# Three stages of attention, soft MoE and an output MLP on one core: first loads, last pair's outputs, last w2, and the first chunk of the last stage in another order

## The reference

```python
q_pool = q.reshape(B, H, S // 2, 2, D).mean(axis=3)          # 576 queries of each head
scores = scale * q_pool @ k.T ; attn = softmax(scores) ; x = attn @ v
...
logits = x @ phi                                              # x (2304, 512), phi (512, 32)
d = softmax over tokens ; slot_input = d.T @ x                # 8 experts, 4 slots each
h = np.maximum(slot_input[e] @ w1[e], 0.0) ; slot_out[e] = h @ w2[e]
x = softmax_over_slots(logits) @ slot_out
...
h = x @ w_in ; g = h - np.tanh(h) ; out = g @ w_out           # w_in (512, 2048), w_out (2048, 512)
```

## Time and profile before

| | us |
|---|---|
| median of 3 runs (lowest to highest) | 835.5 (834.91 to 835.62) |
| the profiled execution's own time | 835.48 |
| its span in the trace | 833.7 |
| PE busy in the span | 789.9 (95%) |
| DVE, ACT, POOL busy | 521.4, 504.1, 248.7 |

### The profile page before, as it was taken

The page is one execution under the profiler, slowest core; times in us unless marked ns, Lnnn a source line. Parts: engine busy times, 40 slices in busy tenths (PEclk is TensorE's granted clock), DMA queues, the critical chain, the costliest instruction groups (busy, mean ns, idle before and its releaser), DMA issues. The chain is left out here.

```text
span 833.7 us, 16574 instructions
## 1 busy us (share of the span) xinstructions
PE 789.9 (95%) x5819; PEld 596.7 (72%) x5819; DVE 521.4 (63%) x988; ACT 504.1 (60%) x878; POOL 248.7 (30%) x156
## 2 busy tenths in 40 slices
PE   4899999999999999999999998888879999999998
PEld 3777777777777777777777775644348888888886
DVE  3666766766766766766776674520076766667673
ACT  3676676676676676676666755311196666666662
POOL 2304304404404404403403300000086343434342
PEclk8999999999999999999999999899999999999999
DMA  6453303303303303303303175289920000000000
GB/s 142 145 147 86 84 4 87 85 0 85 85 0 85 85 0 85 85 0 85 85 0 86 65 268 206 98 328 396 387 101 26 13 13 25 25 25 25 25 25 25
DMA packets 83728, 75.49 MB, mean 91 GB/s; under 512 B 42480, under 2 KB 60912, under 8 KB 83696
## 3 DMA queue, kind: packets, MB, share of 16 engines
q1 hardware_dynamic: 81360, 74.47, 27.9%
q10 hardware_dynamic: 2336, 0.59, 0.4%
HBM read 70.32 MB, written 4.72 MB: 90 GB/s over the span
## 5 line engine op out<-in xcount | busy, mean ns | idle before, releaser
L535 ACT ACTIVATE prob<-ps,neg_max 128x512 f32<-128x512 f32 (+1 forms) x144 | 141.5, 983 | 146.7 <-DVE spare L442 145.5
L321 PE MATMUL ps<-ident,prob 128*128 128x128 f32 x1296 | 164.7, 279 | 11.3 <-ACT prob L535 9.3
L321 PEld LDWEIGHTS ps<-ident,prob 128*128 128x128 f32 x1296 | 141.2, 142 | 37.9 <-ACT prob L535 31.5
L337 PE MATMUL ps<-probT,v_nat 128*64 128x256 f32 (+1 forms) x1152 | 153.6, 411 | 0.0
L438 DVE TENSOR_REDUCE part_neg<-ps 128x1 f32<-128x512 f32 x160 | 109.3, 692 | 49.2 <-PE ps L276 41.6
L412 DVE COPY probT<-ps 128x128 f32<-128x128 f32 (+1 forms) x208 | 86.7, 442 | 66.8 <-PE ps L321 63.2
L211 POOL TENSOR_TENSOR kT<-k_raw,ones 128x1152 fp32r<-128x1152 f32 x15 | 31.6, 2107 | 295.1 <-ACT k_raw L507 295.1
L507 ACT ACTIVATE probT<-ps 128x512 f32<-128x512 f32 x192 | 106.3, 602 | 21.8 <-PE ps L321 21.3
L337 PEld LDWEIGHTS ps<-probT,v_nat 128*64 128x64 f32 x1152 | 77.1, 136 | 50.9 <-issue 3.2
L276 PE MATMUL ps<-kT,qT_hi 64*128 64x512 f32 (+1 forms) x768 | 109.0, 360 | 2.4 <-DVE qT_lo L429 2.4
L1042 PE MATMUL ps<-w_hi,g_even 128*128 128x512 f32 x320 | 102.7, 392 | 2.2 <-POOL g_even L1132 2.1
(11 more groups left out here) (155 smaller groups left out, 1106.0 us busy)
## 6 DMA issues: line engine op xcount, KB each, us to landing
slot<-in_moe_w SPq DMA_DIRECT2D x16, 2048.0 KB, 13.0
v_nat<-in_v SPq DMA_DIRECT2D x16, 576.0 KB, 5.0
k_nat<-in_k SPq DMA_DIRECT2D x30, 288.0 KB, 4.1
q_nat<-in_q SPq DMA_DIRECT2D x32, 256.0 KB, 4.2
out<-res SPq DMA_DIRECT2D x18, 256.0 KB, 2.0
slot<-in_moe_w_in SPq DMA_DIRECT2D x4, 1024.0 KB, 15.6
slot<-in_moe_w_out SPq DMA_DIRECT2D x8, 512.0 KB, 11.7
q_nat_r<-in_q SPq DMA_DIRECT2D x32, 32.0 KB, 3.5
```

The lines of the kernel that those rows point to most:

```text
L321: last = nc.tensor.transpose(dst[:, n * P:(n + 1) * P], prob[h][:, kt * P:(kt + 1) * P], ident[:])
L337: last = nc.tensor.matmul(ps[64 * h:64 * h + D, VBANK, 0:n], v_nat[par][:, h, kt, :], probT[g][:, kt, h, :], start=(kt == 0), stop=(kt == ...
L535: nc.scalar.activation(prob[h][:, 0:first], row[:, 0:first], ACT.Exp, bias=neg_max[:, j:j + 1], scale=-1.0, accum_out=sums).then_inc(exp_b ...
```

## The change

Five edits, here with the lines that matter.

First pair's loads: each of the two queues, SP and ACT, issues one k DMA and then one q DMA.

```diff
+                first = isinstance(n, int) and n == 0
+                wait(sp, ktr_full, n * 2)
+                load_k(sp, n, (0,) if first else (0, 1))
                 wait(sp, q_sum, 2 * n)
...
+                load_q(sp, n, (0,) if first else (0, 1))
                 sp.wait_ge(rest_zero, 1)
...
-            load_k(act, 0)
+            load_k(act, 0, (1,))
+            load_q(act, 0, (1,))
```

```diff
+            def last_pv(p, par):
+                pe.wait_ge(first_evac, tiles_of(p, ROUNDS))
+                pv(p, par, 1, 0, 8, False)
+                pe.wait_ge(second_a, (p + 1) * ROUNDS)
+                pe.wait_ge(second_b, doubles_of(p, ROUNDS))
+                pv(p, par, 1, 8, 16)
+                pe.wait_ge(third_evac, tiles_of(p, ROUNDS))
+                pv(p, par, 1, 16, 18)
...
                 if last:
-                    wait(pe, first_evac, tiles_of(p, ROUNDS))
-                    turn_out(p, 0)
-                    pv(p, par, 1, 0, len(PV_ORDER))
-                    pe.wait_ge(out_evac, p * 2 + 1)
+                    pe.wait_ge(first_evac, tiles_of(p, ROUNDS) - 1)
+                    turn_out(p, 0, 0)
+                    last_pv(p, par)
                     turn_out(p, 1)
...
+                    if last and r == ROUNDS - 1:
+                        empty_v(dve, nc.vector.tensor_copy, p, 0)
...
-                    empty_v(p, 0)
-                    empty_v(p, 1)
+                    empty_v(act, copy, p, 1)
```

```diff
-                for q in (1, 3):
-                    part = u4[q * NS:(q + 1) * NS, n * BANK:(n + 1) * BANK]
-                    ins = nc.vector.tensor_tensor(part, ps[q * NS:(q + 1) * NS, u_bank(n), :], part.bitcast(F32), ALU.subtract)
-                ins.then_inc(u_lo, 1)
+                part = u4[P // 2:P, n * BANK:(n + 1) * BANK]
+                nc.vector.tensor_tensor(part, ps[P // 2:P, u_bank(n), :], part.bitcast(F32), ALU.subtract).then_inc(u_lo, 1)
...
+                    if e == E - 1 and f % (FTE // len(last_w2)) == 0:
+                        pe.wait_ge(last_w2[f // (FTE // len(last_w2))], 16)
```

```diff
-                        for n in ((0, 1), (2,), (3,), ())[b]:
-                            u_high(n)
-                            if n == 0:
-                                for k in (0, 1, 2):
-                                    w_high(k)
+                        if b == 0:
+                            u_high(0)
+                            w_high(0)
+                            u_high(1)
+                        elif b == 1:
+                            u_high(2)
...
+                    if is_first(c) and b:
+                        high(c, par, b - 1)
+                        if b == 1:
+                            u_high(3)
...
-                        for k in ((3,), (4, 5), (6, 7), ())[b]:
+                        for k in ((1,), (2, 3), (4, 5), (6, 7))[b]:
                             w_high(k)
...
-                        for n in ((0, 1, 2, 3), (4, 5), (), (6, 7))[b]:
+                        for n in ((0, 1), (2,), (4,), (6,))[b]:
                             w_low(n)
...
-                        for n in ((0, 1), (2,), (3,), ())[b]:
+                        for n in ((0, 1), (2, 3), (), ())[b]:
                             u_low(n)
...
+                    if is_first(c) and b:
+                        w_low(2 * b + 1)
...
-                pe.wait_ge(gl_done, c * BLOCKS + b + 1)
+                block = range(b * FB, (b + 1) * FB)
+                both_high_first = is_first(c)
                 pe.wait_ge(gh_done, c * BLOCKS + b + 1)
...
+                    for ft in block:
+                        product(par, i, ft, g_hi, w_hi)
...
+                        product(par, i, ft, g_hi, w_lo)
+                    if not both_high_first:
+                        project_low(c, par, b, i)
+                if both_high_first:
+                    for i in range(TPC):
+                        project_low(c, par, b, i)
```

More of the change, by code:

```diff
@@ L131, in attention, with load_k, load_q @@
         block = ctx.enter_context(nc.Block())
-        def load_k(eng, n):
-            for h in range(2):
+        def load_k(eng, n, heads=(0, 1)):
+            for h in heads:
                 eng.dma_start(k_nat[:, :, h, :], k_src[:, bass.ds(n * 2 + h, 1), :].rearrange("p o (t d) -> p (o t) d", d=D)).then_inc(k_in, 16)
+        def load_q(eng, n, heads=(0, 1)):
+            for h in heads:
+                eng.dma_start(q_nat[:, h].rearrange("p t a d -> p t (a d)"), q_main[:, bass.ds(n * 2 + h, 1)].rearrange("p o t e -> p (o t) e")).then_inc(q_in, 16)
         @block.sync
@@ L322, in turn_prob, with pv @@
                     last.then_inc(ptr_full, 1)
-            def pv(p, par, g, lo, hi):
+            def last_pv(p, par):
[6 more added lines that the diff above has]
+                pv(p, par, 1, 16, 18)
+            def pv(p, par, g, lo, hi, whole=True):
                 n = GN[g]
@@ L328, in pv @@
                     wait(pe, pv_evac, p * 2 + g)
+                if lo == 0 and whole:
                     rounds = MIX + 1 if g == 0 else ROUNDS
@@ L412, in evac, with empty_v @@
             return copy(probT[g][:, k0:k1, h, col:col + P], src.rearrange("p (c q) -> p c q", c=n))
+        def empty_v(eng, copy, p, g):
+            eng.wait_ge(pv_done, p * 2 + g + 1)
+            wait(eng, otr_full, p * 2 + g - 1)
+            copy(outT[g][:], ps[:, VBANK, 0:GN[g]]).then_inc(pv_evac, 1)
         def group_free(eng, p, r):
@@ L549, in body @@
                     if r == 0 and not first:
-                        empty_v(p - 1, 0)
+                        empty_v(act, copy, p - 1, 0)
                     for h in range(heads_of(r)):
@@ L565, in body @@
                     if r == MIX - 1 and not first:
-                        empty_v(p - 1, 1)
+                        empty_v(act, copy, p - 1, 1)
                     if r != MIX:
@@ L1028, in hidden, with product @@
                 last.then_inc(m_full, 1)
+            def product(par, i, ft, a, w, stop=False):
+                return nc.tensor.matmul(ps[:, 2 * HB + i, :], a[par][:, ft * CW + i * P:ft * CW + (i + 1) * P], w(ft),
+                                        start=(ft == 0 and a is g_hi and w is w_hi), stop=stop)
             def project(c, par, b):
-                pe.wait_ge(gl_done, c * BLOCKS + b + 1)
+                block = range(b * FB, (b + 1) * FB)
+                both_high_first = is_first(c)
                 pe.wait_ge(gh_done, c * BLOCKS + b + 1)
@@ L1037, in project, with project_low @@
                         wait(pe, o_evac[i], c)
-                    for ft in range(b * FB, (b + 1) * FB):
+                    for ft in block:
+                        product(par, i, ft, g_hi, w_hi)
                         if i == 0 and ft % PF == 0:
-                            pe.wait_ge(wl_done, ft // PF + 1)
-                        for k, (a, w) in enumerate(((g_hi, w_hi), (g_hi, w_lo), (g_lo, w_hi))):
-                            last = nc.tensor.matmul(ps[:, 2 * HB + i, :], a[par][:, ft * CW + i * P:ft * CW + (i + 1) * P], w(ft),
-                                                    start=(ft == 0 and k == 0), stop=(ft == FT - 1 and k == 2))
-                    if b == BLOCKS - 1:
-                        last.then_inc(o_full, 1)
+                            n = ft // PF
+                            if n % 2 and n > 1:
+                                pe.wait_ge(wl_dve, n // 2)
+                            else:
+                                pe.wait_ge(wl_pool, n // 2 + 1 + (n > 0))
+                        product(par, i, ft, g_hi, w_lo)
[4 more added lines that the diff above has]
+                        project_low(c, par, b, i)
+            def project_low(c, par, b, i):
+                if i == 0:
+                    pe.wait_ge(gl_done, c * BLOCKS + b + 1)
+                for ft in range(b * FB, (b + 1) * FB):
+                    last = product(par, i, ft, g_lo, w_hi, stop=(ft == FT - 1))
+                if b == BLOCKS - 1:
+                    last.then_inc(o_full, 1)
             def body(c, par):
@@ L1257, in program @@
         w2_in = [sem(f"w2_in{e}") for e in range(E)]
+        last_w2 = [sem(f"last_w2_{n}") for n in range(4)]
         slot = [half(f"slot{n}", n) for n in range(len(SLOTS))]
@@ L1266, in load @@
                              dram["moe_w1"][e].rearrange("(k p) f -> p k f", p=P)).then_inc(w1_in[e], 16)
+            elif e == E - 1:
+                FQ = FE // P // len(last_w2)
+                src = dram["moe_w2"][e].rearrange("(f p) d -> p f d", p=P)
+                for n, landed in enumerate(last_w2):
+                    sp.dma_start(space[e][1].rearrange("p (f d) -> p f d", d=DM)[:, n * FQ:(n + 1) * FQ, :],
+                                 src[:, n * FQ:(n + 1) * FQ, :]).then_inc(landed, 16)
             else:
@@ L1312, in program @@
                   (slot[4], slot[5]), res)
-        experts_mlp(nc, (E, DM, FE, NS, FF, B * SQ), sb, ident, rep, siT, [(space[e], (e, 16)) for e in range(E)], (w1_in, w2_in),
```

(1 more changed line is left out.)

41 lines of the change are left out of this document (18 added, 23 removed).

## The result

| | before | after |
|---|---|---|
| median (lowest to highest), 6 runs each on one chip | 835.85 (834.91 to 836.7) | 831.68 (828.22 to 832.5) |
| ratio to before, 95% interval | | 0.9935 (0.992 to 0.995) |
| the profiled execution's own time | 835.48 | 832.08 |
| its span | 833.7 | 830.3 |

The change makes the kernel 0.65% faster by the ratio, which is 5.4 us of the 835.5 before and gives 830.1; by the two medians it is 4.2 us. The forecast was 7.5, at 828.0. 830.1 lies outside its central band (827.2 to 828.9) and inside its range (825.2 to 830.8) with little to spare; the interval of the ratio reaches from 828.8 to 831.3, beyond the range, and so does the plain median of 831.68. In the experiments the same kernel took 829.69 against 836.55. Why one kernel gives both is the first question for them.

The account below looks back on a forecast made before the run. PE, busy 95% of the span, was taken as the bound through its waits, with DMA then an ACT/POOL hand-over in the second half. Gains 1.1 + 1.0 + 5.4 = 7.5 took 835.5 to 828.0 us; range 825.2 to 830.8.

Parts of the forecast that it names:

- First loads: Kernel start: k lands earlier, q's rest becomes the bound, first scores at 11.9 instead of 13.01; gain 1.1 us, bounds 0 to 2.2.
- rival 3: Slow-clock stretch before the load stream is cut from 6.4 to 3.4, release 1.5 us earlier: 826.5 us; chance 0.20.
- rival 2: Last stage: half clock in blocks 0 and 1, DVE's `w_low` at 2.38; 5.1 us won, 830.4; chance 0.12.
- Last pair: End of attention: DVE copies group 0, so PE turns it without its 1.05 us idle time; 1.0 us taken.
- w2 in quarters, u's low part in one: Last expert: PE reaches `u_part` 1.4 us earlier, but ACT still waits for w_out; costed at 0.
- First chunk: Last stage's first chunk: POOL stops being the chain, ACT is late next, PE reaches chunk 1 earlier; gain 5.4 us.
- the release of `res`: Chunk 1's first `project`: its second tile waits 0.5 us until DVE, done with block 5's g at 638.2 + 0.7, empties it.
- Clock in the last stage: Last stage: full PE clock taken after a 1.7 us idle stretch; half clock for 7 us would cut 5.9 to 3.8.
- (1): Load stream doesn't shift with PE's release, ACT's wait for w_out absorbs 2.1 us: 830.1; chance 0.15 together with (5).
- (4): First chunk: DVE and POOL hold each other up, ending it 3.6 us later than now: 837.0; slower had chance 0.01.
- (5): Loads or last pair don't gain, the k side being no bound: 829 to 830; chance 0.15 together with (1).

Follow-up runs that it names:

- e1_loads_alone: The kernel before with only the new order of the first pair's k and q loads, against the kernel before: median 835.89 us, ratio 0.9992 (0.9979 to 1.0006).
- f2_spin_gating: The changed kernel with unread identity transposes on PE at the start, plus 15 more in gating: 823.79 us, against 826.34 without those 15.

## Why the prediction was right or wrong

**First loads**: the mechanism and its place were right. k landed earlier, the q side took over, and the first scores stood at 11.95 (forecast 11.9). q's rest landed 0.22 later, within what was allowed for. What the step is worth in time no run shows: with filler it was 1.3 at the load of phi in one pair of traces, but other traces with the same start and filler gave anything from 1.3 to -0.5, and `e1_loads_alone` has an interval that holds no change. The step that failed is the tacit one behind it, that the first rounds would run as in the profiled execution of before. The bounds of this term were 0 and 2.2; in the profiled execution it was -2.3, as 3.4 us went between the first scores and the load of phi, where the rows have the lengths of half clock. The text priced a better clock here (in the chance of rival 3) and a worse one only for the last stage (rival 2). The half clock at the start was missing, and with it 2 us at the top of the range.

**Last pair**: right in the rows, while the medians (0.24) don't show it alone. 1.0 was taken, with 1.05 as the most it could be; the rows show 1.25 (6.53 to 5.28). The bound was too low, as the idle time of 1.05 is counted from the end of the last transpose in the row (508.99 + 2.19), while without a wait the turn starts 2.02 us behind the start of the 18 transposes and not 2.19 (511.29 to 513.31).

**w2 in quarters, u's low part in one**: right at 0. PE's wait of 1.68 went down to 0.28, and the time did not move.

**First chunk**: the mechanism was right, the size was off: 4.27 for 5.4. POOL stopped being the chain, and ACT became it, as written: ACT's chain to the fourth `high` starts at 26.66 behind `w_high(0)` (forecast 26.4), PE's blocks 0 and 1 begin at 8.73 and 15.04 (forecast 8.42 and 14.87). Chunk 1's first `project` then came at 34.49 and not 33.4: blocks 2 and 3 do tile 0's low part first, since c is a register there, and last 6.50 and 5.95, not 5.5. But the runs show that this is not what cost the microsecond. The term that was mis-sized is the release of `res`. Forecast 638.2 + 0.7, which is 36.7 behind `w_high(0)`, it came at 640.8 (37.4), and with it the 12 products behind took 3.04 and not 2.74. A part of this delay is the three `w_low` on DVE at 1.64 and not 1.22, as the series of block 5 stands behind the last of them; how much is not separated. That the `project` with the wait lasts 5.85 us (637.88 to 643.73 in the timeline), 0.38 over 5.47 with 0.5 forecast, is chance: PE was late by about as much as DVE.

**Clock in the last stage**: full, as taken. `hidden` of block 2 waited 1.65 us for u's low part at 609.9 to 611.5, and the granted clock stayed at 1.00.

**Rivals.** (1) the stream does shift, by `f2_spin_gating`. (2) neither half came: full clock, `w_low` at 1.64. (3) right in kind, but it needs PE to be kept busy; moving all by 2 us did not do it. (4) DVE's `w_low` cost 1.64 where 3.6 was needed to lose the gain, and taking them off DVE loses 3.1. (5) the number came out where rivals 1 and 5 had it (830.1, and 829 to 830): the gain of the loads did not arrive, but through the clock behind the first scores and not through k.

The chances were right on the sign: faster by over 0.2% had 0.97, and the interval is 0.5 to 0.8%. That the number lies inside the range is in part luck: the range was wide enough at the top for other reasons than the one that used it up, and an execution like the median of after (831.68) lies outside.

## What to carry to other kernels

A single profile shows one draw of TensorE's clock at the start and behind every pause, so before a few microseconds are forecast from it, look at the lengths of like rows (here 0.73 or 1.22 us for four products) and leave that much room on both sides. Where PE waits on the path, work that nobody reads can be worth nearly as much as a better order: 43 transposes at the start and 15 in gating gave 5.9 us, the whole reordering some 7. When a bound is taken away, follow each engine that comes after it into the next iteration, down to the buffer's release: two PE waits that looked like the loss were hidden by a later one, for a copy on DVE. And before a difference between two single traces is put down to an edit, look whether it stood there before the edit's place.

## What the runs showed of the hardware that I had not expected

- The same start comes at either clock: in two kernels that are alike up to there, the first four products of 64x512 took 0.73 us and 1.22, with the same start time (13.01).
- The recorded clock of after was 1.00 at 12 to 13 us while the products had the length of half clock; from its first change (26 to 27 us) on record and lengths agree (nine transposes at 26.64 in 2.15 us).
- The stream of DMAs from its first load to `w_high(0)` took 57.9 to 59.1 us in the thirteen traces where `w_high(0)` waited for it, all of the same bytes.
- DVE and POOL cost each other little when both read two operands from SBUF: 1.64 for 1.22 (the 1.22 with one operand from PSUM), and 2.65 for 2.42.
